# Attention in front of two expert layers: the output turned back a pair later in the score banks, and q, k and v loaded over all partitions at once

## The chip, the cores and the metric

One core of one Trainium2 chip runs the whole program in one launch. The metric is the device time of that launch in microseconds, as the median of several runs.

## What is computed

Attention with a learned position bias feeds a mixture of experts and then a gated feed-forward layer. Only the attention matters here:

```python
B, H, S, D = 4, 8, 576, 64
scores = scale * np.matmul(q, k.transpose(0, 1, 3, 2))
x = (np.log1p(np.abs(rel)) / psi_i)[..., None]      # rel = pos_i - pos_j
bias = np.maximum(x @ w1 + b1, 0.0) @ w2            # one value per head, i, j
scores = scores + bias.transpose(2, 0, 1)[None]
attn = np.exp(scores - np.max(scores, axis=-1, keepdims=True))
attn = attn / (np.sum(attn, axis=-1, keepdims=True) + 1e-09)
out = np.matmul(attn, v)
```

The rows of `out` (tokens x 512) then go through `_moe_ref` (8 experts, one per token) and `_moe2_ref`.

## The kernel before

**Stages.** A bias stage computes the bias table (`bias_stage`, up to about 62 us) and stores it to HBM. The attention follows (`front_stages`, to about 364 us), then routing, experts and the feed-forward layer, which the change doesn't touch.

**Pairs and slots.** Attention runs over NPAIR = 16 pairs of heads, pair p having batch p % 4 and head pair p // 4. The 576 query rows of a pair are cut into five slots: 0 to 3 hold 128 rows of either head (two units, h = 0 and 1), and slot 4 (`MIX`) the last 64 rows of both heads in one unit. That is nine units a pair. Each unit passes TensorE (`scores`, line 428, 4 matmuls of 288 columns, 8 for slot 4), VectorE (`add_bias`, line 587, with the row maximum), ScalarE (`exps`, line 653, with the row sum), and VectorE again (`turn`, line 597, a transpose into `pt`). The score banks are `s_ps`, two banks for each h, so the scores of one slot wait for the adds of the slot before (`s_b`).

**The sums.** `values` (line 535) multiplies `pt` by v on TensorE. It needs every transpose of its pair, so it runs one pair later. Its 18 blocks of keys are dealt over slots 0 to 3 of the following pair by `VISITS` (3, 5, 5 and 5 blocks, 16 matmul passes each), behind the scores that TensorE computes one slot ahead. They accumulate in four banks, `o_ps`.

**Out again.** In slot 4 ScalarE copies the sums to `ot` (`keep_out`, line 663, signals `s_oe`), and TensorE multiplies them back to rows = tokens and by the gate weights (`turn_back`, line 556, ten matmul passes, signals `s_bk`). Its output lies in `back_ps`, which are the first two banks of `o_ps`. VectorE divides by the row sums (`normal`, line 614, twice a pair, writes `a_xp`, signals `s_x`) in slot 0 of the next pair. So the next sums, which overwrite these banks, wait for `s_x` (line 542). GpSimd adds the gate logits (`add_logits`, line 499) after `normal`, and SyncE stores the tokens (`store_first`, `store_second`).

**Queues.** All loads and stores here go through SyncE, in written order: q and k of pair p + 2 (`load_qk`), the stores of pair p - 2, new bias tiles in each fourth pair, v of pair p + 1. In pair 0 v of pairs 0 and 1 stands behind q and k of pair 2. q and k must be twice in SBUF (partitions 0 to 63 and 64 to 127), v four times (every 32 partitions), so `load_qk` makes 4 loads and `load_v` 4, each from the same source rows. GpSimd splits q and k of a coming pair in two parts (`split_k`, `split_q`) as soon as the scores that use the same buffer are done. In the bias stage `loads` (line 389) issues q and k of pair 1 in steps 22 and 24.

Of the kernel before, what the change touches and what calls it, by code (L numbers as in the profile page):

```python
# [26 lines left out]
TPP = 9  # L27
# [248 lines left out]
def front_stages(sem, arena, psum, qt, kt, vt, ww, wg, biasd, xd, ident, rt, small):  # L276
# [6 lines left out]
    NG, NK = P // Q, S // Q  # L283
    VISITS = (range(0, 3), range(3, 8), range(8, 13), range(13, NK))
    pt = arena.at("a_pt", [P, 2, NK, 2 * P + Q], arena.PT)
# [19 lines left out]
    o_ps = psum[:, 4:8, :]  # L305
    back_ps = [psum[:, 4, :], psum[:, 5, :]]
    s_init, s_bias = sem("a_init"), [sem(f"a_bias{t}") for t in range(SLOTS)]
# [6 lines left out]

    def load_qk(e, pair, u, halves=(0, 1)):
        for half in (slice(64 * i, 64 * i + 64) for i in halves):
            e.dma_start(qraw[half, u, :, :].rearrange("p a s -> p (a s)"),
                        qt[bass.ds(pair, 1), :, :, :].rearrange("a p h s -> p (a h s)")).then_inc(s_q[u], 16)
            e.dma_start(kraw[half, u, :], kt[bass.ds(pair, 1), :, :].rearrange("a p s -> p (a s)"))\
                .then_inc(s_k[u], 16)  # L320

    def load_v(e, pair, u):
        for g in range(NG):
            e.dma_start(vv[Q * g:Q * g + Q, u, :, :].rearrange("p k d -> p (k d)"),
                        vt[bass.ds(pair, 1), :, :].rearrange("a p n -> p (a n)")).then_inc(s_v[u], 16)

# [9 lines left out]
    def set_constants(e):  # L336
        for u in range(2):
            e.memset(qs[:, u, S:640].bitcast(f32), 0.0).then_inc(s_init, 1)
        e.memset(xw[:, :, :, 64:XW], 0.0).then_inc(s_init, 1)
        for h in range(2):  # L340
            e.tensor_copy(xw[:, :, h, 0:64], ident[:, 64 * h:64 * h + 64].unsqueeze(1).to_broadcast([P, H // 2, 64]))\
                .then_inc(s_init, 1)
        e.wait_ge(s_init, sem.at(s_init, 5))
        e.wait_ge(s_k[0], sem.at(s_k[0], 32))
        e.tensor_copy(khi[:, 0, :], kraw[:, 0, :]).then_inc(s_sp, 1)
        e.wait_ge(s_q[0], sem.at(s_q[0], 32))
        e.tensor_copy(both(0, slice(0, P)), qraw[:, 0, :, :]).then_inc(s_qh, 1)
# [9 lines left out]
    def split_k(e, it, u):  # L357

        pair = it * 2 + u
        e.wait_ge(s_k[u], sem.at(s_k[u], it * 32 + 32))  # L360
        sem.apart(e, it)
# [13 lines left out]
    def split_q(e, it, u):  # L375

        pair = it * 2 + u
        e.wait_ge(s_q[u], sem.at(s_q[u], it * 32 + 32))
        sem.apart(e, it)
# [9 lines left out]
    def loads(e, step):  # L389

        if step in (2, 4, 6, 8):
            small(e, step // 2 - 1)
        if step in (22, 24):
            load_qk(e, 1, 1, (step // 2 - 11,))
        if step in (28, 30):
# [32 lines left out]
    def scores(e, p, u, uses, s, h):  # L428

        unit = p * TPP + 2 * s + h  # L430
        if s == 0 and h == 0:
            split_done(e, p)
        e.wait_ge(s_b, sem.at(s_b, unit if s == 0 and h == 0 else unit - 2 if s == 0 else unit - 1))
        parts = [(0, BLK), (1, S)] if s == MIX else [(h, 704 * h + P * s)]
# [11 lines left out]
    def sync(e):  # L446
# [18 lines left out]
        def pair(p, u, uses):  # L465
            def next_bias(slots):
                if not isinstance(p, int) and u == 1:
                    with e.If(uses % 2 == 1):
                        for s in slots:
                            e.wait_ge(s_b, sem.at(s_b, p * TPP + min(2 * s + 2, TPP)))  # L470
                            sem.apart(e, p)
                            load_bias(e, (p // B + 1) % (H // 2), s)
            next_bias((0,))
            if not (isinstance(p, int) and p >= NPAIR - 2):
                split_done(e, p)
                load_qk(e, p + 2, u)
            if isinstance(p, int) and p == 0:
                load_v(e, 0, 0)
                load_v(e, 1, 1)
            if from_pair(p, 2):  # L480
                store_first(p - 2, u)
                store_second(p - 2, u)
            next_bias(range(1, SLOTS))
            if from_pair(p, 1) and not (isinstance(p, int) and p == NPAIR - 1):
                e.wait_ge(s_o, sem.at(s_o, p))
                sem.apart(e, p)
                load_v(e, p + 1, 1 - u)

        each_pair(e, pair)
# [43 lines left out]
    def tensor(e):  # L533

        def values(p, u, uses, blocks):

            if blocks[0] == 0:
                e.wait_ge(s_v[u], sem.at(s_v[u], (uses + 1) * NG * 16))
                e.wait_ge(s_t, sem.at(s_t, p * SLOTS + SLOTS))
                sem.apart(e, p)  # L540
                if from_pair(p, 1):
                    e.wait_ge(s_x, sem.at(s_x, p * 2))
                    sem.apart(e, p)
# [12 lines left out]
        def turn_back(p):  # L556

            e.wait_ge(s_oe, sem.at(s_oe, p + 1))
            if isinstance(p, int) and p == 0:
                e.wait_ge(s_wg, sem.at(s_wg, 32))  # L560
# [7 lines left out]
        def pair(p, u, uses):  # L568
            for s in range(SLOTS):
# [3 lines left out]
                if exists(np_) and ns != MIX:  # L573
                    scores(e, np_, nu, nuses, ns, 1)
                if s != MIX and from_pair(p, 1):
                    values(p - 1, 1 - u, uses - 1 + u, VISITS[s])
                if s == MIX and from_pair(p, 1):
                    turn_back(p - 1)

        each_pair(e, pair)  # L580
        last = NPAIR - 1
        values(last, 1, NPAIR // 2 - 1, range(NK))
        turn_back(last)

    def vector(e):
# [42 lines left out]
        def pair(p, u, uses):  # L628
            for s in range(SLOTS):
# [3 lines left out]
                if exists(np_) and ns != MIX:  # L633
                    add_bias(np_, nu, nuses, ns, 1)
                if s == 0 and from_pair(p, 2):
                    for half in range(2):
# [1191 lines left out]
```

## Time and profile before

| what | us |
|---|---|
| median of 3 runs | 1098.96 (1096.1 to 1109.04) |
| profiled execution | 1099.54 |
| its span in the profile | 1097.7 |
| TensorE busy | 1014.5 (92% of the span) |
| VectorE busy | 793.3 (72%) |
| ScalarE, GpSimd busy | 411.2, 204.8 |
| mean granted TensorE clock | 0.963 of 2.4 GHz |

Rows of the view by stretch give: the stretch; its length; busy time of PE (TensorE matmuls), PEld (its weight loads), DVE (VectorE), ACT (ScalarE) and POOL (GpSimd), each with its count of instructions; the granted TensorE clock; the mean busy share of the DMA engines; GB/s. Rows of the timeline give: start, duration, engine, line, operation, output <- inputs, and in brackets the idle time before it with what ended it; SPq is SyncE's queue of DMA issues. Rows of waits give: who waited <- for whom: total us, how often, the longest. A matmul's own duration contains its way through the array, and matmuls overlap; how many start in a stretch tells the rate.

### The profile page before, as it was taken

The page shows a single profiled execution, that of the slowest core. Times are in us where ns is not written, and L with a number is a line of the kernel's source. Part 1 is how long each engine was busy: PE and PEld are TensorE (multiplying, and loading weights), DVE is VectorE, ACT ScalarE, POOL GpSimd, SP SyncE. Part 2 cuts the span into 40 slices and gives each one's busy share as a digit, 9 for nine tenths or more (in the row PEclk, how much of TensorE's full clock was granted, in tenths as well). Part 3 has the DMA queues.
Part 4 walks back from the last instruction along what each step waited for, and adds up shares of the span by engine and source line. Part 5 has one row for each costly group of instructions (what it writes and reads, how often), then busy time and mean ns, then how long its engine had stood idle before and what let it go on. Part 6 is the DMA issues. An engine that isn't in the chain of part 4 may idle for free.

```text
span 1097.7 us, 28662 instructions
## 1 busy us (share of the span) xinstructions
PE 1014.5 (92%) x10409; PEld 921.0 (84%) x10410; DVE 793.3 (72%) x1268; ACT 411.2 (37%) x783; POOL 204.8 (19%) x195
## 2 busy tenths in 40 slices
PE   5867778898888999999999999999999999999997
PEld 2346666676777899999999999999999999999996
DVE  8974768777787654774747479878777777777775
ACT  7863444444454334654434244221221212212111
POOL 2044243525360141221212000001010000100101
PEclk9987899989999889999999999999999999999999
DMA  4886688977963573561612170002000100100000
GB/s 148 288 230 141 146 208 170 235 152 160 227 151 67 168 240 117 191 205 61 203 50 88 60 258 2 1 0 80 29 29 0 45 12 0 57 0 0 30 1 29
DMA packets 68078, 117.43 MB, mean 107 GB/s; under 512 B 28384, under 2 KB 39696, under 8 KB 65984
## 3 DMA queue, kind: packets, MB, share of 16 engines
q1 hardware_dynamic: 64000, 103.45, 34.2%
q0 software_dynamic: 4032, 13.37, 3.8%
q8 instruction: 28, 0.46, 0.2%
q14 instruction: 18, 0.15, 0.0%
HBM read 91.41 MB, written 25.40 MB: 106 GB/s over the span
## 4 chain that ended last, share of the span: by engine, by line
PE 84%; issue 4%; DVE 3%; DMA 3%; ACT 3%; DVEq 1%; SPq 0%; ACTq 0%; POOL 0%; POOLq 0%
PE psum L1700 27%; PE psum L1708 13%; PE psum L1213 10%; PE psum L1222 10%; PE psum L551 10%; PE psum L438 8%; DMA bias_ihj<-b_res 2%; PE psum L563 2%; PE psum L1199 1%; DVE a_xp L624 1%; DMA a_v<-v 1%; PE psum L843 1%; ACT b_hid L234 1%; ACT a_ot L667 1%; ACT b_res L244 1%
## 5 line engine op out<-in xcount | busy, mean ns | idle before, releaser
L1655 DVE RECIPROCAL f_eg<-f_eg 128x384 f32<-128x384 f32 x72 | 183.3, 2546 | 0.0
L659 ACT ACTIVATE a_pr<-a_sc,a_nmax 128x576 f32<-128x576 f32 x144 | 110.9, 771 | 151.5 <-DVE a_nmax L593 151.0
L593 DVE CUSTOM_DVE_ANT_0 a_sc<-psum,a_bias 128x576 f32<-128x576 f32 x144 | 105.0, 755 | 75.2 <-PE psum L438 72.4
L551 PE MATMUL psum<-a_pt,a_v 32*64 32x128 f32 (+1 forms) x4608 | 108.8, 316 | 49.3 <-DVE a_xp L624 33.4
L1623 ACT ACTIVATE f_eg<-psum 128x384 f32<-128x384 f32 x72 | 35.4, 492 | 311.9 <-PE psum L1700 311.9
L1700 PE MATMUL psum<-f_x,f_ghi 128*128 (+1 forms) x576 | 147.5, 337 | 0.4 <-DVE f_x L1516 0.4
L1700 PE MATMUL psum<-f_x,f_vhi 128*128 (+1 forms) x576 | 146.1, 334 | 0.0
L551 PEld LDWEIGHTS psum<-a_pt,a_v 32*64 32x64 f32 x4608 | 87.7, 143 | 62.5 <-issue 57.1
L438 PE MATMUL psum<-a_khi,a_qs 128*128 128x288 f32 x320 | 107.7, 354 | 4.3 <-DVE a_nmax L593 4.2
L1700 PEld LDWEIGHTS psum<-f_x,f_ghi 128*128 128x128 f32 x576 | 105.8, 188 | 6.6 <-DVE f_x L1516 0.6
L1592 POOL DMA_INDIRECT out<-f_ob,f_cols x18 | 18.1, 1006 | 465.0 <-ACT f_ob L1609 316.3
L1700 PEld LDWEIGHTS psum<-f_x,f_vhi 128*128 128x128 f32 x576 | 104.0, 188 | 0.0
L605 DVE STREAM_TRANSPOSE a_pt<-a_pr 128x576 f32<-128x576 f32 x144 | 103.9, 756 | 0.0
L438 PE MATMUL psum<-a_klo,a_qs 128*128 128x288 f32 x320 | 98.0, 324 | 0.0
L1700 PE MATMUL psum<-f_x,f_glo 128*128 (+1 forms) x288 | 97.1, 337 | 0.0
L1700 PE MATMUL psum<-f_x,f_vlo 128*128 (+1 forms) x288 | 96.2, 334 | 0.0
L1651 DVE TENSOR_SCALAR f_eg<-f_eg 128x384 f32<-128x384 f32 x72 | 26.4, 367 | 88.5 <-ACT f_eg L1623 88.5
L438 PEld LDWEIGHTS psum<-a_khi,a_qs 128*128 128x128 f32 x320 | 68.8, 215 | 22.9 <-issue 17.6
L1222 PE MATMUL psum<-e_hhi,e_w2hi 128*128 128x288 f32 x288 | 87.4, 303 | 0.0
L1213 PE MATMUL psum<-e_xhi,e_w1hi 128*128 128x288 f32 x288 | 86.7, 301 | 0.0
L1708 PE MATMUL psum<-f_ohi,f_alo 128*128 128x512 f32 x216 | 85.4, 396 | 0.0
L1708 PE MATMUL psum<-f_olo,f_ahi 128*128 128x512 f32 x216 | 85.3, 395 | 0.0
(235 smaller groups left out, 2162.7 us busy)
## 6 DMA issues: line engine op xcount, KB each, us to landing
a_v<-v SPq DMA_DIRECT2D x64, 288.0 KB, 5.4
e_raw<-ew SPq DMA_DIRECT2D x16, 1024.0 KB, 5.2
bias_ihj<-b_res SPq DMA_DIRECT2D x36, 288.0 KB, 2.8
a_qraw<-q SPq DMA_DIRECT2D x32, 288.0 KB, 7.4
a_kraw<-k SPq DMA_DIRECT2D x32, 288.0 KB, 8.1
a_bias<-bias_ihj SPq DMA_DIRECT2D x16, 576.0 KB, 6.2
xn_t<-e_yn SPq DMA_DIRECT2D x8, 576.0 KB, 3.1
x_tokens<-a_xp SPq DMA_DIRECT2D x64, 64.0 KB, 6.3
```

Of the source, the lines that this page charges most:

```text
L438: mm = e.matmul(s_ps[:, h, half, 0:HALF], qs[:, u, c:c + P], k[:, u, a * S + half * HALF:a * S + (half + 1) * HALF], start=(i == 0), stop= ...
L551: mm = e.matmul(o_ps[64 * h:64 * h + 64, g, to:to + n], vv[rows, u, k, 64 * h:64 * h + 64], pt[rows, u, k, first:first + n], start=(k == 0 ...
L593: e.tensor_tensor_reduce(sc[:, h, :].rearrange("p (a s) -> p a s", a=2), s_ps[:, h, :, 0:HALF], bias[:, 2 * s + h, :].rearrange("p (c s) - ...
L605: t = e.transpose(pt[:, u, :, at:at + Q], pr[:, w, S * h:S * h + S].rearrange("p (k q) -> p k q", q=Q))
L659: mm = e.activation(pr[:, w, S * h:S * h + S], sc[:, h, :], ACT.Exp, bias=nmax[:, h:h + 1], scale=-1.0, accum_out=sums[:, u, 2 * s + h:2 * ...
L1213: mm = e.matmul(bank[:, 0:BT], w[:, k, :], x[:, u, k, :], start=(k == 0 and n == 0), stop=(k == KD - 1 and n == 2))
L1222: mm = e.matmul(banks.y[:, k, 0:BT], w[:, k * P:(k + 1) * P], h[:, f % 3, :], start=(f == 0 and n == 0), stop=(f == KF - 1 and n == 2))
L1623: e.activation(self.eg[:, k % 2, :], self.g_ps[k % 2][:, 0:CHUNK], ACT.Exp, scale=-1.0).then_inc(self.s_e, 1)
L1651: e.tensor_scalar(x, x, 1.0, None, ALU.add).then_inc(self.s_c, 1)
L1655: e.reciprocal(x, x).then_inc(self.s_c, 1)
L1700: mm = e.matmul(acc[:, 0:CHUNK], a, b, start=(q == 0 and i == 0), stop=(q == KD - 1 and i == 2))
L1708: mm = e.matmul(self.o_ps[t], x, y, start=(f == 0 and i == 0), stop=(f == KFF - 1 and i == 2))
```

## The change

- `back_ps` moves from `o_ps` to the h = 1 score banks. `turn_back(p - 2)` runs in slot 3 of pair p, between the scores of slot 4 and the sums, no longer `turn_back(p - 1)` in slot 4. It waits also for `normal` of the pair before it and for the add of slot 3, h = 1. The last two turns stand behind the loop.
- `normal(p - 2)` moves on VectorE from slot 0 to slot 3 of pair p. The scores of slot 0, h = 1 of the next pair wait for it (`s_x`).
- `values` waits for ScalarE's copy (`s_oe`) in place of `s_x`.
- `VISITS` deals 5, 5, 5 and 3 blocks.
- q, k and v are replicated on the host, and each is one load over 128 partitions; the semaphores count 16 in place of 32 or 64. q and k of pair 1 are both issued in step 22.
- SyncE's order: v of pair 0 ahead of q and k of pair 2; the stores of pair p - 2 at the end of pair p, behind v and all bias tiles, and the bias tile of slot 4 behind v.

```diff
-    VISITS = (range(0, 3), range(3, 8), range(8, 13), range(13, NK))
+    VISITS = (range(0, 5), range(5, 10), range(10, 15), range(15, NK))
-    back_ps = [psum[:, 4, :], psum[:, 5, :]]
+    back_ps = [s_ps[:, 1, half, :] for half in range(2)]
-    def load_qk(e, pair, u, halves=(0, 1)):
-        for half in (slice(64 * i, 64 * i + 64) for i in halves):
-            e.dma_start(qraw[half, u, :, :].rearrange("p a s -> p (a s)"),
-                        qt[bass.ds(pair, 1), :, :, :].rearrange("a p h s -> p (a h s)")).then_inc(s_q[u], 16)
...
+    def load_qk(e, pair, u):
+        e.dma_start(qraw[:, u, :, :].rearrange("p a s -> p (a s)"),
+                    qt[bass.ds(pair, 1), :, :].rearrange("a p n -> p (a n)")).then_inc(s_q[u], 16)
+        e.dma_start(kraw[:, u, :], kt[bass.ds(pair, 1), :, :].rearrange("a p n -> p (a n)")).then_inc(s_k[u], 16)
     def load_v(e, pair, u):
-        for g in range(NG):
-            e.dma_start(vv[Q * g:Q * g + Q, u, :, :].rearrange("p k d -> p (k d)"),
-                        vt[bass.ds(pair, 1), :, :].rearrange("a p n -> p (a n)")).then_inc(s_v[u], 16)
+        e.dma_start(vv[:, u, :, :].rearrange("p k d -> p (k d)"),
+                    vt[bass.ds(pair, 1), :, :].rearrange("a p n -> p (a n)")).then_inc(s_v[u], 16)
@@ loads @@
-        if step in (22, 24):
-            load_qk(e, 1, 1, (step // 2 - 11,))
+        if step == 22:
+            load_qk(e, 1, 1)
@@ scores @@
+        if s == 0 and h == 1 and from_pair(p, 3):
+            e.wait_ge(s_x, sem.at(s_x, p * 2 - 4))
@@ sync, pair @@
             next_bias((0,))
+            if isinstance(p, int) and p == 0:
+                load_v(e, 0, 0)
             if not (isinstance(p, int) and p >= NPAIR - 2):
                 split_done(e, p)
                 load_qk(e, p + 2, u)
             if isinstance(p, int) and p == 0:
-                load_v(e, 0, 0)
                 load_v(e, 1, 1)
-            if from_pair(p, 2):
-                store_first(p - 2, u)
-                store_second(p - 2, u)
-            next_bias(range(1, SLOTS))
+            next_bias(range(1, MIX))
             if from_pair(p, 1) and not (isinstance(p, int) and p == NPAIR - 1):
                 e.wait_ge(s_o, sem.at(s_o, p))
                 sem.apart(e, p)
                 load_v(e, p + 1, 1 - u)
+            next_bias((MIX,))
+            if from_pair(p, 2):
+                store_first(p - 2, u)
+                store_second(p - 2, u)
@@ values @@
                 if from_pair(p, 1):
-                    e.wait_ge(s_x, sem.at(s_x, p * 2))
+                    e.wait_ge(s_oe, sem.at(s_oe, p))
@@ turn_back @@
             e.wait_ge(s_oe, sem.at(s_oe, p + 1))
+            e.wait_ge(s_x, sem.at(s_x, p * 2))
+            e.wait_ge(s_b, sem.at(s_b, min((p + 3) * TPP - 1, NPAIR * TPP) if isinstance(p, int) else (p + 3) * TPP - 1))
@@ tensor, pair @@
+                if s == MIX - 1 and from_pair(p, 2):
+                    turn_back(p - 2)
                 if s != MIX and from_pair(p, 1):
                     values(p - 1, 1 - u, uses - 1 + u, VISITS[s])
-                if s == MIX and from_pair(p, 1):
-                    turn_back(p - 1)
...
         last = NPAIR - 1
+        turn_back(last - 1)
         values(last, 1, NPAIR // 2 - 1, range(NK))
         turn_back(last)
@@ vector, pair @@
-                if s == 0 and from_pair(p, 2):
+                if s == MIX - 1 and from_pair(p, 2):
                     for half in range(2):
                         normal(p - 2, u, uses - 1, half)
@@ kernel @@
-        "q": np.ascontiguousarray(qp), "k": np.ascontiguousarray(kp.reshape(NPAIR, D, 2 * S)), "v": np.ascontiguousarray(vp),
+        "q": np.tile(qp.reshape(NPAIR, D, 2 * S), (1, 2, 1)), "k": np.tile(kp.reshape(NPAIR, D, 2 * S), (1, 2, 1)), "v": np.tile(vp, (1, 4, 1)),
```

## Rows read from the trace of the kernel before

**Rows 1.** Busy time by stretch: pair 1, pair 3, eleven pairs, two single pairs.

```profile
83.24:107.94 24.70, 18.90 (x338) 16.14 (x339) 12.39 (x28) 8.37 (x21) 10.19 (x6) 0.76 0.60 131
...
129.65:151.15 21.50, 14.22 (x338) 11.92 (x339) 13.92 (x32) 8.33 (x22) 8.10 (x6) 1.00 0.93 251
...
151.15:339.85 188.70, 160.76 (x3719) 138.25 (x3718) 150.28 (x342) 91.92 (x231) 82.11 (x69) 0.92 0.77 176
...
184.89:200.75 15.86, 13.41 (x338) 11.51 (x338) 13.46 (x32) 8.26 (x21) 7.61 (x5) 1.00 0.76 161
...
218.51:237.29 18.78, 16.31 (x339) 14.09 (x339) 13.72 (x32) 8.41 (x22) 7.62 (x5) 0.83 0.73 156
```

**Rows 2.** Waits from 151.15 to 339.85 us.

```profile
POOL a_khi L367 <- PE psum L438: 87.2, 10, 10.5
DVE a_sc L593 <- PE psum L438: 36.4, 53, 2.1
...
PE psum L551 <- DVE a_xp L624: 27.7, 12, 2.7
```

**Rows 3.** Timeline around the start of the sums of one pair.

```profile
198.29 0.29 PE L438 MATMUL psum<-a_klo,a_qs 128*128 128x288 f32 x1
...
199.64 0.96 DVE L624 TENSOR_TENSOR a_xp<-psum,a_rinv 128x288 f32<-128x288 f32 x2
...
200.75 1.70 PE L551 MATMUL psum<-a_pt,a_v 32*64 32x160 f32 x48 [2.17 <-DVE a_xp L624]
...
202.79 0.44 PE L438 MATMUL psum<-a_klo,a_qs 128*128 128x288 f32 x1
```

**Rows 4.** Timeline of slots 2 to 4 of that pair.

```profile
206.14 0.40 PE L438 MATMUL psum<-a_khi,a_qs 128*128 128x288 f32 x1
...
207.17 0.76 DVE L593 CUSTOM_DVE_ANT_0 a_sc<-psum,a_bias 128x576 f32<-128x576 f32 x1 [0.19 <-PE psum L438]
...
207.40 1.64 PE L551 MATMUL psum<-a_pt,a_v 32*64 32x160 f32 x80
...
207.85 0.75 DVE L593 CUSTOM_DVE_ANT_0 a_sc<-psum,a_bias 128x576 f32<-128x576 f32 x1
...
208.97 0.40 PE L438 MATMUL psum<-a_khi,a_qs 128*128 128x288 f32 x1
...
210.57 0.76 DVE L593 CUSTOM_DVE_ANT_0 a_sc<-psum,a_bias 128x576 f32<-128x576 f32 x1 [0.61 <-PE psum L438]
...
212.34 0.60 ACT L667 ACTIVATE a_ot<-psum 128x512 f32<-128x512 f32 x1
...
213.46 1.49 PE L563 MATMUL psum<-a_xw,a_ot 128*128 x10 [0.28 <-ACT a_ot L673]
...
214.69 0.39 PE L438 MATMUL psum<-a_khi,a_qs 128*128 128x288 f32 x1
```

**Rows 5.** Busy time by stretch: q, k, v loads; bias tile loads.

```profile
70.00:83.00 13.00, 7.00 (x26) 5.82 (x24) 9.90 (x23) 5.91 (x14) 4.54 (x3) 0.63 1.01 225
...
207.50:211.50 4.00, 4.00 (x164) 3.62 (x168) 3.39 (x9) 1.68 (x5) 0.95 (x1) 1.00 1.09 331
```

**Rows 6.** Timeline: v of pairs 0 and 1, and the first sums.

```profile
71.90 4.12 SPq L324 DMA_DIRECT2D a_v<-v  x8
...
76.91 0.77 DVE L605 STREAM_TRANSPOSE a_pt<-a_pr 128x576 f32<-128x576 f32 x1
...
83.24 1.91 PE L551 MATMUL psum<-a_pt,a_v 32*64 32x160 f32 x48 [4.89 <-DMA a_v<-v]
```

**Rows 7.** Timeline: a stall in pair 1; a copy in the bias stage.

```profile
95.25 0.81 PE L551 MATMUL psum<-a_pt,a_v 32*64 32x128 f32 x9 [3.00 <-issue]
...
51.49 0.74 ACT L244 ACTIVATE b_res<-psum,b_invp 128x576 f32<-128x576 f32 x1 [1.85 <-DMA bias_ihj<-b_res]
```

**Rows 8.** DMA issues of the page: count, KB each, us to landing.

```profile
a_kraw<-k SPq DMA_DIRECT2D x32, 288.0 KB, 8.1
```

**Rows 9.** Groups by line, 151.15 to 339.85 us: busy us, mean ns.

```profile
L370 POOL TENSOR_TENSOR a_klo<-a_kraw,a_khi 128x1152 fp32r<-128x1152 f32 x10 | 26.5, 2650 | 1.8 <-POOL a_khi L367 1.8
```

More of the change, by code:

```diff
@@ L313, in front_stages @@
         sem.loop("a_" + n) for n in ("s", "b", "e", "t", "o", "oe", "bk", "r", "x"))
-    def load_qk(e, pair, u, halves=(0, 1)):
-        for half in (slice(64 * i, 64 * i + 64) for i in halves):
-            e.dma_start(qraw[half, u, :, :].rearrange("p a s -> p (a s)"),
-                        qt[bass.ds(pair, 1), :, :, :].rearrange("a p h s -> p (a h s)")).then_inc(s_q[u], 16)
-            e.dma_start(kraw[half, u, :], kt[bass.ds(pair, 1), :, :].rearrange("a p s -> p (a s)"))\
-                .then_inc(s_k[u], 16)
+    def load_qk(e, pair, u):
+        e.dma_start(qraw[:, u, :, :].rearrange("p a s -> p (a s)"),
+                    qt[bass.ds(pair, 1), :, :].rearrange("a p n -> p (a n)")).then_inc(s_q[u], 16)
+        e.dma_start(kraw[:, u, :], kt[bass.ds(pair, 1), :, :].rearrange("a p n -> p (a n)")).then_inc(s_k[u], 16)
     def load_v(e, pair, u):
-        for g in range(NG):
-            e.dma_start(vv[Q * g:Q * g + Q, u, :, :].rearrange("p k d -> p (k d)"),
-                        vt[bass.ds(pair, 1), :, :].rearrange("a p n -> p (a n)")).then_inc(s_v[u], 16)
+        e.dma_start(vv[:, u, :, :].rearrange("p k d -> p (k d)"),
+                    vt[bass.ds(pair, 1), :, :].rearrange("a p n -> p (a n)")).then_inc(s_v[u], 16)
     def load_bias(e, hp, s):
@@ L343, in set_constants @@
         e.wait_ge(s_init, sem.at(s_init, 5))
-        e.wait_ge(s_k[0], sem.at(s_k[0], 32))
+        e.wait_ge(s_k[0], sem.at(s_k[0], 16))
         e.tensor_copy(khi[:, 0, :], kraw[:, 0, :]).then_inc(s_sp, 1)
-        e.wait_ge(s_q[0], sem.at(s_q[0], 32))
+        e.wait_ge(s_q[0], sem.at(s_q[0], 16))
         e.tensor_copy(both(0, slice(0, P)), qraw[:, 0, :, :]).then_inc(s_qh, 1)
@@ L359, in split_k @@
         pair = it * 2 + u
-        e.wait_ge(s_k[u], sem.at(s_k[u], it * 32 + 32))
+        e.wait_ge(s_k[u], sem.at(s_k[u], it * 16 + 16))
         sem.apart(e, it)
@@ L377, in split_q @@
         pair = it * 2 + u
-        e.wait_ge(s_q[u], sem.at(s_q[u], it * 32 + 32))
+        e.wait_ge(s_q[u], sem.at(s_q[u], it * 16 + 16))
         sem.apart(e, it)
@@ L537, in values @@
             if blocks[0] == 0:
-                e.wait_ge(s_v[u], sem.at(s_v[u], (uses + 1) * NG * 16))
+                e.wait_ge(s_v[u], sem.at(s_v[u], (uses + 1) * 16))
                 e.wait_ge(s_t, sem.at(s_t, p * SLOTS + SLOTS))
```

## The prediction

> **What bounds the kernel now.** I read the page first, for the stages and the lines that cost most. The change touches only the attention part, from about 60 to 364 us, so the argument is about that part. The busy time by stage comes next, cut where the value sums of each pair start. In 151.15 to 339.85 us, eleven pairs, TensorE is busy 160.8 of 188.7 us and VectorE 150.3: nearly level, and neither is full; their mean clock is 0.92 [rows 1]. One pair costs 188.7 / 11 = 17.15 us on average. Pairs differ by clock: one with a granted clock of 1.00 took 15.86 us, one with 0.83 took 18.78 [rows 1]. The waits of the same stretch name the gap: TensorE's value sums waited 27.7 us in 12 places, 2.3 us a pair, for VectorE's write of a_xp (line 624, `normal`) [rows 2]. VectorE itself waits 36.4 us for scores, so it has slack too, and GpSimd waits 87.2 us, 8.7 a pair [rows 2]. The timeline shows the gap in one pair: the last score matmul starts at 198.29, `normal` runs from 199.64, the sums begin at 200.75 after 2.17 us of idle TensorE, and right behind this gap a score matmul takes 0.44 us where it took 0.29 before it: the clock fell to the half level [rows 3].
>
> **Part 1: sums wait for the copy alone.** The back-turn's output leaves banks 4 and 5, so the sums of pair p need only ScalarE's copy of pair p-1 (`s_oe`). That copy follows the end of the sums by 0.5 us and takes about 1 us (from 212.34 in this pair) [rows 4], while the sums are some 3 us away behind 16 score matmuls. The 2.3 us wait goes. What is late next has to be walked, since VectorE is nearly full.
>
> Steps, all at clock 1.00 [rows 4]: a group of 8 score matmuls to the sums behind it 1.26 us (206.14 to 207.40), to another group some 0.2 less, 1.05; 80 sums 1.57 (207.40 to 208.97), 48 sums about 1.05; ten back-turn matmuls 1.2 (213.46 to 214.69); scores to the first bias add 1.03 (206.14 to 207.17), for the one unit of slot 4 1.60 (208.97 to 210.57); adds 0.68 apart (207.17 to 207.85); two transposes 1.36 (VectorE's 13.46 us of a pair [rows 1] less 9 adds, `normal` and 0.3 of reciprocals, over 9, twice); the two `normal`s 0.96 [rows 3].
>
> **Part 2: the back-turn a pair later, in the score banks.** It moves from slot 4 to slot 3, between the scores of slot 4 and 48 sums. Its input was copied a pair ago, so the wait for `s_oe` (about 0.3 us of idle now) is gone. Its new wait, for the add of slot 3 half 1, ends some 0.7 us before it is asked, because the slot 4 scores (1.26 us) stand in front. `normal` moves on VectorE behind the slot 4 add. Behind it stand the transposes of slot 3 (nobody needs them for 3 us) and the first add of the next pair. The scores of the next pair's second half now wait for `normal` (`s_x`); it ends about as the first half starts, 0.5 us before the second half is asked.
>
> Walk, 0 being where TensorE starts the next pair's slot 0: VectorE is still busy until 1.0, first add at 1.03, second 1.71, transpose of slot 4 from 2.39 to 3.1. TensorE has issued slot 0 by 1.05 and waits for the first add: slot 1 scores at about 1.95 (a new idle of 0.9 us that the back-turn covered before), second half 2.6, sums of slot 0 (80 now) 3.3 to 4.9, slots 1 and 2 with 1.26 + 1.57 each to 10.5, slot 4 scores to 11.75, back-turn to 12.95, 48 sums to 14.1. VectorE: slot 4 add at 12.1, `normal` 12.8 to 13.8, transposes to 15.15, which is 1.0 into the next pair: the walk closes at 14.2 us. The floors lie just below: VectorE has 9 adds (6.1), 9 transposes (6.2), `normal` 0.9, reciprocals 0.3 = 13.5 us. The same walk for the kernel before gives 15.9 against 15.86 measured [rows 1], so I add only 0.1: 14.3 us at clock 1.00, a gain of 1.55 a pair, not 2.3.
>
> **The clock.** A pair of 17.15 us on average against 15.86 at clock 1.00 loses 1.3 us to stretches at the half level (1.2 GHz) [rows 1]. The idle of 2.17 us before them becomes 0.9 plus two pauses of 0.1 to 0.2. I take it that three quarters of this loss go: the average pair is then 14.3 + 0.3 = 14.6. Eleven pairs: 11 x (17.15 - 14.6) = 28 us. With no such gain it is 11 x 1.55 = 17 us; with all of it 31.
>
> **Part 3: loads over all partitions.** Bytes stay the same: 4 loads of 288 KB for v and 4 for q and k a pair become 3 of 1.18 and 0.59 MB. SyncE issues 3 instead of 8 at some 0.5 us, 2.5 us saved on a queue with room. The rate: the q, k and v loads of 70 to 83 us move 225 GB/s with the engines full, the bias loads over 128 partitions 331 [rows 5]. So between none and a third of the transfer time is saved. In a steady pair it is hidden either way: a pair moves about 2.6 MB (161 GB/s x 15.86 us [rows 1]), 11.4 us at 225 GB/s, and each load has a pair's time to land. It is worth 0 there. The Trainium skill, "SBUF — State Buffer", section on the DMA port swizzle, has 64 partitions reach only half of the ports (196 against 328 GB/s at 1 MiB); this agrees with these two windows, and by it the v load takes about 3.6 us.
>
> **Part 4: v of pair 0 first in the queue.** Now SyncE issues it from 71.90, behind four q and k loads, and TensorE waits 4.89 us, until 83.24, while the last transpose that the sums need starts at 76.91 and ends at 77.68 [rows 6]. Issued at 69.3, 1.18 MB at even 225 GB/s take 5.2 us, with 2 us around it 76.6, before TensorE is free (83.24 - 4.89 = 78.35). The whole 4.9 us go.
>
> **First pairs, end, other queues.** 83.24 to 151.15, three pairs of 24.7 to 21.5 us [rows 1], takes 67.9 us, with stalls that no semaphore explains, 3.00 us in the first [rows 7]; I keep them. Two waits for `normal` there (some 2.3 each) go and pair 1 loses its back-turn (1.5), but the new wait stands against them and a half clock stays in places: -6 us. At the end pair 15 gains a back-turn (+1.2) and values(15) no longer waits for `normal` (-1.0): 0. Bias stage: q and k of pair 1 come as one burst at step 22; a copy waits 1.85 us for a store queued behind these loads now [rows 7]; I take -0.5, bounds +1 and -2. SyncE's stores now stand at the end of a pair and delay the next q and k issue to about 4.5 us into it; with today's landing of 8.1 us [rows 8] they are there at 13.5. GpSimd is held at `add_logits` until `normal` of slot 3 is done: its split starts 2.6 us later, at 15, takes two subtractions of 2.65 us [rows 9] and two casts of about 1.1, some 8 with the pauses, and ends at 23 where it is needed at 28.5. Cost 0 while that slack of 5 us holds.
>
> Sum: -28 - 4.9 - 6 + 0 - 0.5 = -39.4 us. The profiled execution took 1099.5 us (span 1097.7), 0.6 above the median shown: 1099.5 - 39.4 = 1060.1, or 1059.6 against the median. I say 1060.
>
> **Rivals.** (a) The clock is not given back: half-clock stretches stay as they are. For it: they may depend on the whole mix of small pieces, and the slot boundary still has pauses. Then 17 + 4.9 + 4 = 26: 1073. Chance 0.2. (b) VectorE or TensorE doesn't keep the walk: VectorE would be 95% busy, and each handover that runs 0.3 us late five times a pair costs 1.5 us, which eats the gain; what stays is pair 0's v and a little clock: 1085. Chance 0.1. (c) The other side: TensorE gets the half clock more often, because the scores of slots 0 and 1 now come in four short pieces with pauses. A pair at 0.83 took 18.78 us and one at 1.00 15.86 [rows 1], so 0.1 of mean clock costs 1.7 us. A pair of 14.3 is back at 17.15 when its mean clock is 0.83 (now 0.92); at 0.75 it costs 18.6, 11 x 1.4 = 16 us more than now, and less the 9 of the start the kernel takes 1107. Against it: the pauses are shorter than today's. Chance 0.03. (d) Slower by the queue: q and k behind the stores. It decides only if landing takes 18 us instead of 8, then each us costs 15 us in all. Chance 0.02.
>
> **Numbers.** The forecast's own range, 1049 to 1068, has 0.65. The low end takes all of the clock, 14.1 a pair and stalls of the first pairs partly covered; reaching into (a) gives 1049 to 1078 for 8 in 10. Two per cent, about what can be told from no change, is 22 us: below 1077 lies the forecast, (a) nearly whole, 0.85; within 2% 0.12; slower 0.03.
>
> **What would show it.** TensorE has no wait for L624 before the sums; it has waits of about 0.9 us before score matmuls for VectorE's add; pairs of 14.2 to 14.8 us with clock above 0.95; VectorE above 13 us of each; the first sums near 78.4 us; q, k, v packets at over 300 GB/s; GpSimd waits for `normal` and not for scores. It is wrong if pairs stay above 15.5 at clock 1.00 (the walk), if clock stays at 0.9 (the clock step), or if TensorE waits for `a_ql` or a DMA at a pair's start (the queues).

## The result, and the profile after

| | us |
|---|---|
| before, median of 4 runs | 1100.96 (1096.1 to 1109.04) |
| changed, median of 4 runs | 1048.57 (1046.72 to 1052.59) |
| ratio, with its 95% interval | 0.952 (0.946 to 0.959) |
| span of the changed kernel's profile | 1046.9 (before: 1097.7) |

The direction was as forecast, and so was the mechanism in the steady pairs; but the gain is 52 us where 39 were forecast, and the time lies 0.4 us under the low end of the range (1049). The surplus comes from the first three pairs, for a reason that the forecast hadn't.

Busy time by stretch of the changed kernel, cut like [rows 1] where the sums of a pair start: pairs 1, 2 and 3, then eleven pairs. Columns as before.

```profile
80.53:94.39 13.86, 12.84 (x329) 10.61 (x329) 12.06 (x30) 8.27 (x21) 11.65 (x7) 0.99 0.51 192
94.39:113.04 18.65, 15.61 (x338) 13.10 (x339) 14.04 (x32) 8.33 (x21) 6.27 (x5) 0.91 0.35 125
113.04:129.11 16.07, 14.09 (x339) 11.75 (x339) 13.66 (x32) 8.38 (x22) 8.57 (x6) 1.00 0.91 313
129.11:288.06 158.95, 149.14 (x3719) 128.06 (x3719) 149.61 (x342) 91.14 (x230) 86.35 (x70) 1.00 0.64 211
```

Eleven pairs take 158.95 us where [rows 1] have 188.70, 14.45 a pair, at a granted clock of 1.00 where it was 0.92. Pair 1 takes 13.9 us where it took 24.7.

Waits of the changed kernel in its steady pairs, 131.46 to 290.57 us:

```profile
POOL r_part L508 <- DVE a_xp L628: 65.9, 11, 6.6
...
PEld psum L437 <- DVE a_nmax L597: 10.3, 11, 1.0
...
PE psum L437 <- DVE a_nmax L597: 7.8, 11, 0.7
...
POOL a_khi L364 <- PE psum L437: 2.0, 5, 0.4
```

The wait of the sums for a_xp, 27.7 us in [rows 2], is gone. In its place stand eleven waits of TensorE for VectorE's first add of a slot 0: 0.7 us a pair for its matmuls, 0.9 for its weight loads. GpSimd waits for `normal` (now line 628), not for scores.

The start of the attention, where [rows 6] and [rows 7] have a wait of 4.89 us for v and a copy that waits 1.85 us; and the stalls of pairs 2 and 3. Timeline of the changed kernel:

```profile
80.53 1.73 PE L552 MATMUL psum<-a_pt,a_v 32*64 32x160 f32 x80
...
55.12 0.74 ACT L244 ACTIVATE b_res<-psum,b_invp 128x576 f32<-128x576 f32 x1 [4.55 <-DMA bias_ihj<-b_res]
...
100.72 0.96 PE L552 MATMUL psum<-a_pt,a_v 32*64 32x128 f32 x30 [2.08 <-issue]
...
124.52 0.77 PE L552 MATMUL psum<-a_pt,a_v 32*64 32x128 f32 x23 [1.02 <-issue]
```

Nothing waits for v. The copy in the bias stage waits 4.55 us, so the attention begins later. And the stalls without a releaser before the sums, up to 3.0 us each before, are 2.08 and 1.02.

Below, "the stalls" of a kernel are all waits of TensorE's matmuls without a releaser (`<-issue`) of 0.3 us or more in pairs 1 to 3, added up: 9.95 us before (3.00, 2.37, 2.40 and 2.18) and 3.1 in the changed kernel. Pauses of 0.2 us, which every steady pair of the changed kernel has too, are not counted; some of the texts written before a run count them or set the stalls of the changed kernel at 4.1 to 4.5.

**The ledger.** As marks I use the nine-column reciprocal of VectorE (`inverse`), which every pair has once in slot 0, so that all kernels can be cut alike:

| stretch | before | changed | moved | forecast |
|---|---|---|---|---|
| to the mark of pair 1 | 80.4 | 82.7 | +2.3 | -0.5 |
| three pairs | 71.6 | 48.8 | -22.9 | -10.9 (v 4.9, rest 6) |
| eleven pairs | 188.9 | 159.1 | -29.8 | -28 |
| the rest | 756.7 | 756.3 | -0.4 | 0 |
| sum | | | -50.8 | -39.4 |

So most of the miss is in one row: 12 us too little in the first three pairs, and 2 in the eleven, with 3 us of the other sign in the bias stage. In the three pairs, cut as in [rows 1], TensorE's busy time fell from 50.0 to 42.5 us (1.4 of it the turn-back that pair 1 no longer has; granted clock 0.86 before, 0.96 after). The stalls fell by 6.9 us, and the rest is waits for v and for `normal`.

### The profile page after: what moved, and what is told of

Read it like the earlier page. It is cut to its first block, busy times and chain, and to the rows that moved or that the text cites. A ratio compares the mean times of both kernels' runs of the same rounds, so it can differ in the third digit from the quotient of the medians.

```text
span 1046.9 us, 28553 instructions
## 1 busy us (share of the span) xinstructions
PE 993.2 (95%) x10409; PEld 901.3 (86%) x10410; DVE 791.9 (76%) x1268; ACT 410.0 (39%) x783; POOL 203.8 (19%) x195
## 4 chain that ended last, share of the span: by engine, by line
PE 68%; DVE 2%; issue 1%; POOL 1%; ACT 1%; DMA 0%; POOLq 0%; DVEq 0%
PE psum L1704 28%; PE psum L1712 14%; PE psum L1217 11%; PE psum L1226 11%; PE psum L1203 1%; PE psum L552 1%; PE psum L437 1%; DVE f_eg L1659 0%; PE psum L1265 0%; PE psum L566 0%; DMA e_xin<-x_tokens,e_col 0%; PE psum L847 0%; DVE r_inq L962 0%; POOL e_xin L1169 0%; POOL e_col L1165 0%
## 5 line engine op out<-in xcount | busy, mean ns | idle before, releaser
L437 PE MATMUL psum<-a_khi,a_qs 128*128 128x288 f32 x320 | 101.1, 336 | 13.8 <-DVE a_nmax L597 13.8
L1596 POOL DMA_INDIRECT out<-f_ob,f_cols x18 | 18.2, 1009 | 464.9 <-ACT f_ob L1613 316.9
L552 PE MATMUL psum<-a_pt,a_v 32*64 32x128 f32 (+1 forms) x4608 | 98.9, 294 | 8.3 <-issue 8.3
L552 PEld LDWEIGHTS psum<-a_pt,a_v 32*64 32x64 f32 x4608 | 79.6, 131 | 20.1 <-issue 17.9
L437 PEld LDWEIGHTS psum<-a_khi,a_qs 128*128 128x128 f32 x320 | 62.4, 195 | 34.6 <-DVE a_nmax L597 17.9
L437 PE MATMUL psum<-a_klo,a_qs 128*128 128x288 f32 x320 | 90.9, 304 | 0.0
```

The costliest lines, as they stand in the source:

```text
L437: mm = e.matmul(s_ps[:, h, half, 0:HALF], qs[:, u, c:c + P], k[:, u, a * S + half * HALF:a * S + (half + 1) * HALF], start=(i == 0), stop= ...
L552: mm = e.matmul(o_ps[64 * h:64 * h + 64, g, to:to + n], vv[rows, u, k, 64 * h:64 * h + 64], pt[rows, u, k, first:first + n], start=(k == 0 ...
```

## Experiments: which part brings what

All kernels below start from the kernel before or from the changed one, and were timed beside the kernel before on the same chip; the ratio to it has a 95% interval where it is given. The chips differ from one group of kernels to another, so differences of medians between groups are good to a few microseconds only, and stalls come from one profile of each kernel.

**The turn-back alone.** From the changed kernel, the loads and v's place are put back:

```diff
-        e.dma_start(vv[:, u, :, :].rearrange("p k d -> p (k d)"), ...
+        for g in range(NG):
+            e.dma_start(vv[Q * g:Q * g + Q, u, :, :].rearrange("p k d -> p (k d)"), ...
...
-            if isinstance(p, int) and p == 0:
-                load_v(e, 0, 0)
...
```

> The turn-back part alone: banks, waits, block deal, place of the turn and of the stores as in the changed kernel; q, k and v still loaded in 4 + 4 pieces, v of pair 0 behind q and k of pair 2. Theory 1 (the first three pairs gained 19 us, 13 more than forecast, because TensorE no longer waits for v and so keeps its clock, and because stalls without a releaser depend on when the code is reached): steady pairs 14.5 us, the wait for v of 4.9 us and the slow clock of pair 1 stay, so first sums at about 83 us and pairs 1 to 3 about 58 to 60 us; time 1063 to 1068. Theory 2 (long packets of the old loads hold up the loading of code and the clock follows): the same 14.5 in the steady pairs where no code is loaded, but the stalls without a releaser in pairs 1 to 3 stay at 10 us; time also about 1065, told apart by these stalls.

Measured: 1069.93 us, ratio 0.970 (0.962 to 0.978), some 2 us above both theories. Three pairs take 65.4 us and not 58 to 60, eleven pairs 162.5 (14.8 each), then a last pair 17.3 us where the changed kernel has 13.1. The stalls stay, 10.3 us where the kernel before has 9.95. That is what theory 2 says: the turn-back leaves them alone. Its own -6 us in the first three pairs (71.6 to 65.4) are of the size of the forecast.

**The loads alone.** The kernel before with the new load form and nothing else:

```diff
-        for g in range(NG):
-            e.dma_start(vv[Q * g:Q * g + Q, u, :, :].rearrange("p k d -> p (k d)"), ...
+        e.dma_start(vv[:, u, :, :].rearrange("p k d -> p (k d)"), ...
...
```

> The kernel before with each of q, k and v as one load over 128 partitions (q and k of pair 1 both in step 22), nothing else. Theory 1: steady pairs unchanged at 17.1 us, the wait for v falls from 4.9 to about 1 us since the same bytes land at 330 instead of 225 GB/s, the bias stage is 2 us longer as in the changed kernel; stalls in pairs 1 to 3 stay near 10 us; time 1093 to 1098. Theory 2: the stalls fall from 10 to 3 us as in the changed kernel; time 1084 to 1089.

Measured: 1079.3 us, ratio 0.983 (0.974 to 0.991). By the ratio that is 19 us (10 to 28) less than before, by the medians 22 to 24; and it is 5 less than even theory 2 said. Busy time by stretch: its first three pairs, then its steady ones.

```profile
79.61:133.25 53.64, 43.89 (x1015) 37.53 (x1015) 41.29 (x94) 25.71 (x66) 28.62 (x17) 0.94 0.62 219
...
133.25:320.83 187.58, 159.63 (x3718) 137.44 (x3718) 150.27 (x342) 91.85 (x231) 82.16 (x69) 0.93 0.50 175
```

The steady pairs cost 17.05 us as before (17.15). Nearly all is won in the first three, 53.6 us for 67.9, and ahead of them, where the first sums start 3.6 us earlier. The wait of TensorE's first sums there (its timeline):

```profile
79.61 1.09 PE L548 MATMUL psum<-a_pt,a_v 32*64 32x160 f32 x48 [1.39 <-DMA a_v<-v]
```

That is 3.5 us of the 4.9 us wait for v, without moving v in the queue. The stalls fall to 1.8 us, at a pace of the pairs that is no faster than before. Theory 2 holds in this: the load form governs them. How it does so is the question of the next three kernels.

**v first, alone.** The kernel before, `load_v(e, 0, 0)` ahead of `load_qk` in pair 0.

> The kernel before with v of pair 0 issued ahead of q and k of pair 2, in the old pieces, nothing else. Theory 1: the wait of 4.9 us goes and pair 1 keeps more of its clock (24.7 us before, 20 to 21 after); time 1090 to 1093. Rival: only the wait goes, or the wait for v moves to q and k of pair 2, which come later: time 1096 to 1101.

Measured: 1096.1 us, ratio 0.9965 (0.992 to 1.001), so the time alone doesn't tell. The trace does: the first sums start at 77.93 us with no wait, the three pairs take 64.3 us (7.4 less), and the stalls are 10.7 us, one of them 4.5. So the wait went as forecast, and the stalls stayed with the old load form; the time is that of the rival. The three parts overlap: alone they take 6.3, 18.2 and 7.4 us from the three pairs, together 22.9.

**Why the load form matters to the stalls.** The trace lists instructions among the traffic of the core's 16 DMA engines, in packets of 16 KB on a queue of their own (28 of them in the kernel before). One of them is in the microsecond from 92 us of the kernel before, when the q, k, v transfers run dry (queue: packets, MB, share of the engines' time):

```profile
q8 instruction: 1, 0.02, 7.6%
```

It begins at 92.49 us and takes 1.22; TensorE stands still from 92.25 to 95.25 [rows 7]. In the changed kernel the packet that comes next after the bias stage begins at 85.09 us, and TensorE works on without a stall until 98.6. In the steady pairs, 170 to 260 us, no kernel's trace has an instruction packet, and such stalls don't occur there. The question is whether the code waits for the length of the data burst (theory L) or for single packets of data ahead of it (theory S). A packet of v, 9216 B, takes 656 ns on the average in the kernel before and 424 ns in the changed one; one of q or k, 4608 B, 297 and 213 ns.

Longer bursts, new form: v's first 16 blocks loaded a second time, into spare space.

```diff
+        e.dma_start(v_more[:, u, :, :].rearrange("p k d -> p (k d)"),
+                    vt[bass.ds(pair, 1), :, 0:(NK - 2) * P].rearrange("a p n -> p (a n)")).then_inc(s_v[u], 16)
```

> The changed kernel with 16 of v's 18 blocks loaded a second time into spare space behind each v load (1.05 MB more a pair, packets of 8192 B over all partitions, and the sums wait for both), so that the transfers in front of the code's packets last as long as in the kernel before while their shape stays the new one. Theory L (a code packet comes to its turn when the queued data ahead of it is gone, so the stalls follow the length of the bursts): the stalls without a releaser in pairs 1 to 3 rise from 4.5 to 8 to 11 us, pairs 1 to 3 take 54 to 58 us in place of 48.8; steady pairs, which load no code, stay at 14.4 to 14.8; time 1053 to 1060. Theory S (what matters is the time of a single packet, 656 ns in the old form against some 400): stalls stay below 5.5 us and the time below 1051.

Measured: 1055.91 us, ratio 0.962 (0.955 to 0.969), in the range of theory L. But the stalls are 5.4 us for 3.1, under the 8 to 11 of theory L, and three pairs take 52.0 us for 48.8 where it said 54 to 58. Steady pairs are 14.56 us for 14.46. The profiled execution, 1051.6 us, was the fastest of four. So longer bursts cost something, 2.3 us of it in stalls, and this kernel decides for neither theory.

Shorter packets, old form: each old load cut in two column halves.

```diff
         for g in range(NG):
-            e.dma_start(vv[Q * g:Q * g + Q, u, :, :].rearrange("p k d -> p (k d)"),
+            for c in range(2):
+                e.dma_start(vv[Q * g:Q * g + Q, u, 9 * c:9 * c + 9, :].rearrange("p k d -> p (k d)"),
...
```

> The kernel before with every load of q, k and v cut in two halves of its columns: same 32 or 64 partitions, same bytes, packets of 4608 and 2304 B in place of 9216 and 4608, twice as many loads. Theory L: the port or the engines stay as slow, the bursts as long, the stalls without a releaser in pairs 1 to 3 stay at 9 to 11 us, time 1096 to 1106. Theory S: single packets are half as long, the stalls fall to 5 us or less, time 1085 to 1092.

Measured: 1093.35 us, ratio 0.994 (0.991 to 0.998). Busy time by stretch while the first loads run, and the one stall that is left, in the timeline:

```profile
60.00:83.00 23.00, 14.77 (x72) 11.63 (x72) 16.93 (x39) 15.28 (x33) 12.07 (x10) 0.76 0.79 214
```

```profile
96.31 0.81 PE L553 MATMUL psum<-a_pt,a_v 32*64 32x128 f32 x9 [3.52 <-issue]
```

The rate is as low as in [rows 5] and the wait for v as long (4.79 us), so the bursts are as long. The packets of v now take 294 ns, and the stalls fall from 9.95 to 3.5 us, which speaks for theory S. But they fall by the three of pairs 2 and 3. The stall of pair 1, in front of the same nine matmuls as in [rows 7], is 3.52 us where it was 3.00, and its instruction packet begins at 93.56 us, again in the microsecond in which the data run dry: this one was not helped by shorter packets, as theory L says. The time, too, lies between the two theories; the three pairs (65.1 us) kept their slow clock (0.84). So neither theory holds for all stalls.

Shorter packets, new form, on top of the better bias stage shown below:

> The changed kernel with q and k of pair 1 at the start (e4_qk1_early) and every load of q, k and v cut in two column halves, still over all 128 partitions: packets of 4608 and 2304 B at the new rate, some 200 and 100 ns each. Theory S (the code's packets wait behind single packets of data): the stalls without a releaser in pairs 1 to 3 fall from 4.1 to 1 to 2.5 us, pairs 1 to 3 from 47.8 to 44 to 46 us, time 1 to 4 us below e15_early_again. Theory M (below some 400 ns a packet no longer counts; what is left of the stalls is the distance from one code packet to the next): stalls stay at 3.5 to 4.5, no difference beyond 1 us.

Measured: 1043.87 us (1040.83 to 1045.25), beside 1042.3 for the same kernel with whole packets; stalls 3.6 us beside 2.5. Packets of v take 211 ns in place of some 420, and nothing is won: that is theory M, as far as the new form goes.

Shown is, then, that the load form decides: stalls of 9.95, 10.3 and 10.7 us with the old one in whole packets, 0 to 5.4 with the new one. By which way is open: size and number of the packets, the rate and the length of the burst all change with it. When TensorE gets to a piece of code counts as well: the kernel below that makes the sums wait in each pair has the new loads and no stall at all in pairs 1 to 3. The 2 to 5 us that are left in the others are not explained by any run, and differences of a microsecond between single profiles carry no weight.

## Experiments: the steady pairs and the clock

**The wait put back.** In the changed kernel the sums wait again for VectorE, now for its transposes of slot 0, which stand about where `normal` stood:

```diff
                     e.wait_ge(s_oe, sem.at(s_oe, p))
                     sem.apart(e, p)
+                if not isinstance(p, int) or p < NPAIR - 1:
+                    e.wait_ge(s_t, sem.at(s_t, p * SLOTS + SLOTS + 1))
+                    sem.apart(e, p)
```

> The changed kernel, but the sums wait again for VectorE in slot 0: for the transposes of slot 0 of the following pair, behind two adds and in the place where `normal` stood (1.4 us of VectorE in place of 1.0). This gives the wait of 2.2 to 2.7 us back without moving anything. Theory A (this wait was the cost, and it also pulled the clock down): TensorE waits some 2.5 us a pair before the sums, granted clock of the steady pairs falls from 1.00 to 0.90 to 0.97, and pairs take 16.5 to 17.5 us; time 1076 to 1092. Theory B (the clock depends on the mix, not on this gap): clock stays at 1.00, pairs take 15.8 to 16.4; time 1065 to 1075.

Measured: 1107.62 us, ratio 1.007 (1.004 to 1.010): this wait alone costs more than the whole change brought. Busy time of eleven pairs, waits of the same stretch, and the timeline after one such wait:

```profile
137.69:346.48 208.79, 170.25 (x3718) 146.43 (x3719) 150.50 (x341) 91.72 (x231) 84.18 (x70) 0.86 0.50 160
...
PE psum L555 <- DVE a_pt L612: 30.9, 11, 2.9
```

```profile
156.10 2.98 PE L555 MATMUL psum<-a_pt,a_v 32*64 32x160 f32 x80 [2.73 <-DVE a_pt L612]
...
159.41 0.44 PE L437 MATMUL psum<-a_klo,a_qs 128*128 128x288 f32 x1
...
161.18 1.64 PE L555 MATMUL psum<-a_pt,a_v 32*64 32x160 f32 x80
```

The wait is 2.8 us a pair. A pair takes 18.98 us and not 14.5 + 2.8: behind the wait the 80 sums take 2.98 us in place of 1.64 and score matmuls start 0.24 us apart in place of 0.13, the half level (1.2 GHz), until about 161 us. So a wait of 2.8 us costs 4.5. This is theory A, and more than its upper end of 17.5 us a pair, which had only the mean clock of the kernel before in it. Here the clock falls behind each of the eleven waits. In the kernel before, the wait for `normal` was 2.0 to 2.7 us, and the clock fell behind nine of twelve. Its length doesn't say which: the two longest, 2.70 and 2.67 us, left the clock up, and the shortest, 1.98 us, didn't. The longest, in the timeline of the kernel before:

```profile
151.15 1.07 PE L551 MATMUL psum<-a_pt,a_v 32*64 32x160 f32 x48 [2.70 <-DVE a_xp L624]
...
152.53 0.29 PE L438 MATMUL psum<-a_khi,a_qs 128*128 128x288 f32 x1
```

**Which engine sets the pair.** Two kernels with work left out, of which only the length of the pairs is read:

```diff
-            ops = [(a, c, k) for a, c in parts for k in (khi, klo)]
+            ops = [(a, c, k) for a, c in parts for k in ((khi, klo) if s == 0 else (khi,))]
```

> The changed kernel without the low part of k in the scores of slots 1 to 4 (16 of 40 score matmuls a pair left out, 2.1 us of TensorE), to see which engine sets a steady pair. If VectorE is the bound, pairs stay at 14.1 to 14.5 us; if TensorE is, they fall to 12.4 to 12.9; if both in turn as in the walk, about 13.7. Only the length of the pairs is read, since what comes behind depends on values that this changes.

```diff
-                t = e.transpose(pt[:, u, :, at:at + Q], pr[:, w, S * h:S * h + S].rearrange("p (k q) -> p k q", q=Q))
+                n_k = NK if p_first(p) else NK // 2
+                t = e.transpose(pt[:, u, 0:n_k, at:at + Q], pr[:, w, S * h:S * h + n_k * Q].rearrange("p (k q) -> p k q", q=Q))
```

> The changed kernel with only the first half of each transpose from pair 2 on (some 3 us of VectorE a pair left out), the other side of the same question. If VectorE is the bound, pairs fall to about 13.3 us, where TensorE's own work ends it; if TensorE is, they stay at 14.4. Only the length of the pairs is read.

Measured, by the marks: 13.2 to 13.4 us in most pairs without these scores (13.5 on the average of ten), and 14.1 to 14.4 (mean 14.2) with half transposes, against 14.46. Each kernel ran once. Busy time of ten pairs of the first and eleven of the second:

```profile
144.16:279.60 135.44, 119.59 (x3236) 97.92 (x3243) 132.03 (x312) 82.98 (x210) 77.40 (x66) 0.97 0.69 227
```

```profile
129.57:285.50 155.93, 148.27 (x3719) 127.50 (x3718) 121.32 (x342) 91.58 (x232) 84.56 (x70) 1.00 0.66 214
```

2.6 us of VectorE less a pair (149.6 to 121.3 us over eleven pairs) gains 0.3 us; 2.1 us of TensorE less gains 0.9 (1.1 in most pairs), and then VectorE is busy 132.0 of 135.4 us. So TensorE sets the pair, and VectorE stands about 1 us behind it. The 0.7 us wait of TensorE for the first add is not a wait for a busy VectorE: it is the way score, add, next score, and it stays with half transposes.

## Experiments: the bias stage, and a faster version

**q and k of pair 1 at the start.** In the changed kernel the copy behind step 22 waits 4.55 us. Both loads go to the start of the stage, where the DMA engines are busy 38% of the first 10 us and then idle until the first store at 13 us:

```diff
-        if step == 22:
-            load_qk(e, 1, 1)
...
-                              {"first loads": lambda e: load_qk(e, 0, 0), "loads": loads,
+                              {"first loads": lambda e: (load_qk(e, 0, 0), load_qk(e, 1, 1)), "loads": loads,
```

> The changed kernel with q and k of pair 1 issued right behind those of pair 0 at the start of the bias stage, where the DMA engines are idle until the first store at 13 us, in place of step 22. In the changed kernel one copy of the bias stage waits 4.55 us for a store queued behind these two loads (kernel before: 1.85 and 1.1 in two places). If those loads are the cause, the bias stage ends 4 to 5 us earlier, at about 60.5 us in place of 65, and the time is 1043 to 1045. Rival: the stage's stores fill the DMA engines anyway, and the waits stay at other steps; time 1048.

Measured: 1043.17 us (1042.75 to 1043.54), ratio 0.9475 (0.941 to 0.954). The first mark stands at 78.1 us in place of 82.7, and no copy waits more than 0.2 us for a store. All of the 5 us came.

**The two loads two steps apart.** q in step 22, k in step 24:

> The changed kernel with q of pair 1 in step 22 and k of pair 1 in step 24, each still one load over 128 partitions. If the burst of 1.18 MB in one step makes the stage 2.3 us longer than before, half of it goes: first score add of the attention at about 63 us in place of 64.3, time 1046 to 1047. Rival: the wait comes from the fence of all stores ahead of the bias tile of step 26 and any load ahead of it costs the same: no change, 1048.5.

Measured: 1045.93 us (1045.69 to 1046.99); the first mark is at 80.9, and the copies wait 3.1 us in four places, none over 1.3. So the burst in one step cost 2 us of its own, and any load in that stretch the rest.

**Sums in slot 4.** The wait for the first add can be filled. On top of the kernel with the early loads, one block of sums in slot 4, and then two (the edit shown):

```diff
-    VISITS = (range(0, 5), range(5, 10), range(10, 15), range(15, NK))
+    VISITS = (range(0, 5), range(5, 10), range(10, 14), range(14, 16), range(16, NK))
...
-                if s != MIX and from_pair(p, 1):
+                if from_pair(p, 1):
```

> The changed kernel with q and k of pair 1 at the start (as e4_qk1_early, 1043.2 us) and the last of the 18 blocks of sums moved from slot 3 to slot 4, behind the scores of the next pair's slot 0, where TensorE waits 0.7 to 1.0 us a pair for VectorE's first add. The block takes about 0.35 us and fills part of that wait; the copy by ScalarE starts later but is not asked for another 1.5 us. Expected: pairs 14.1 to 14.3 in place of 14.55, time 1037 to 1041. Rival: the scores of half 1 then wait for `normal`, or the sums for the copy, and nothing is gained: 1043.

> The same with two blocks in slot 4 and two in slot 3 (5, 5, 4, 2, 2). By the walk the wait for the first add is filled whole, but the sums of the next pair start only when the copy is done, about 1.6 us behind the last block, where the scores between last 1.3: pairs 13.9 to 14.2, time 1035 to 1040. Rival: VectorE, 13.5 us busy a pair, sets the pace with its order, and the time equals that of e11_one_block_slot4 within 2 us.

Measured: 1044.15 us (1042.74 to 1047.36) with one, 1041.37 (1041.1 to 1042.34) with two; both expectations were missed. With one, the steady pairs are 14.27 us by the marks, as expected, but the three pairs take 50.1 us for 47.8 and the last one 15.0 for 13.0, and nothing is gained. With two, the steady pairs take 14.07 us, 0.4 less, some 4 us in all. Part of it is lost again near the end: the last pair takes 15.2 us in place of 13.0, by a stall without a releaser, in the timeline of the kernel with two blocks:

```profile
284.70 1.82 PE L550 MATMUL psum<-a_pt,a_v 32*64 32x128 f32 x39 [2.42 <-issue]
```

With half packets as well, beside the kernel with the early loads on the same chip:

> Both at once: two blocks of sums in slot 4 (e12_two_blocks_slot4) and half packets over all partitions. If the parts add up, 2 us from the blocks and what e13_early_half_packets gains: 1036 to 1041; rival: the stall near the end of the loop (2.4 us in e12_two_blocks_slot4) stays and the time is within 1 us of 1041.

> e4_qk1_early unchanged, on the same chip as the two beside it, so that one or two microseconds between them can be told: 1042 to 1044.

Measured: 1039.96 us (1039.5 to 1041.63) and 1042.3 (1042.06 to 1042.69). The ratios to the kernel before are 0.946 (0.937 to 0.954) and 0.9475 (0.939 to 0.956). The fastest version is 2.3 us under its neighbour, about 9 under the changed kernel (timed on another chip), and its four runs lie wholly below the neighbour's. The half packets have no share in it that can be told.

## Why the prediction was right and where it failed

- **The wait of the sums.** Right: it went, and the turn-back part alone brought 33 us (ratio 0.970).
- **The walk.** 14.3 us at clock 1.00 were forecast, 14.45 measured. The pause of TensorE in front of slot 1 was given as 0.9 us and is 0.7 to 0.9. The floors were read well: VectorE's 13.5 us is about where the pairs stop (13.2 to 13.4) when TensorE has less to do, and it lies 1 us below the pair, which TensorE sets.
- **The clock.** The step was right, its size too small: three quarters of 1.3 us a pair were taken, all of it came (1.00). Together with the walk, whose 14.3 us was 0.15 too short, the steady term is 29.8 for 28; that it came so near is in part two errors of opposite sign. And the reason given, that the idle of 2.17 us shrinks, holds for this change as a whole (the wait put back brought the half level back), though the length of a wait doesn't decide it.
- **v first.** Right: no wait for v, in the changed kernel and alone.
- **Loads over all partitions, "worth 0 there".** "There" is a steady pair, and there the 0 was right at the old pace (17.05 us for 17.15); at the new pace the old form costs 3.4 us in eleven pairs, with waits for a bias tile and for k. What failed is that the sum has no term for the load form anywhere else: alone it brings some 20 us, and about as much, with v's place, on top of the turn-back, nearly all in the first three pairs. The waits of VectorE and GpSimd of the turn-back alone, 146.65 to 309.17 us:

```profile
POOL a_khi L367 <- DMA a_kraw<-k: 8.3, 2, 4.2
...
DVE a_sc L599 <- DMA a_bias<-bias_ihj: 5.2, 4, 1.6
```

- **"Stalls that no semaphore explains: I keep them."** This step failed, and most of the miss lies in it: they were carried over without a reason. They depend on the form of the loads, and fell from 9.95 to 3.1 us. With them and the wait for v went the half level of the first pairs (0.76 and 0.84 to 0.99 and 0.91), for which the sum had no term either: TensorE's busy time in the three pairs is some 6 us less by it. The -6 us given for these pairs is what the turn-back brings alone (-6.3). The 12 missing come with the load form, as the kernel with the loads alone shows; how they divide between stalls and clock isn't shown by a run of its own.
- **The bias stage.** -0.5 with bounds +1 and -2; measured +2.3, outside. The burst was seen, but its cost was weighed against the wait there was (1.85 us), not against the fence: SyncE waits in step 26 for earlier stores to land before it issues the bias tile, and some of them stand behind 1.18 MB. In the changed kernel it has issued the last store by 50.3 us and the tile only at 55.03 (before: 49.4 and 51.40); its timeline:

```profile
55.03 0.34 SPq L331 DMA_DIRECT2D a_bias<-bias_ihj  x1
```

- **GpSimd and the stores.** Right: GpSimd waits for `normal`, 6 us a pair, and nobody for GpSimd.

## What to carry to other kernels

Read the stalls without a releaser in a trace against the DMA packets of that moment: where code is still being loaded, as in the pairs before a loop and its first pass, the form of the data loads beside it can be worth more than the length of their transfers. Don't carry such stalls over as a constant. A wait of TensorE is worth more than its length when the clock falls behind it, here 4.5 us for 2.8, so it is to be removed first. And look for idle time of the DMA engines (here before the first store at 13 us) before putting a load into a stretch in which stores pace the work.

## What was not expected of the hardware

- A packet of v, 9216 B, took 656 ns in loads over 32 partitions and 424 ns over 128; the changed kernel's stretch from 80 to 83 us moved 415 GB/s, where [rows 5] have 225. The Trainium skill, "SBUF — State Buffer", section on the DMA port swizzle, has 32 or 64 partitions reach 8 of the 16 ports and 128 all of them; these two rates agree with it.
- Loads over 128 partitions in place of 32 and 64, and nothing else, took the stalls in code loading from 9.95 to 1.8 us. Halving packets in the old form, at an unchanged rate, took away three of the four and left that of pair 1 (3.52 us). The Trainium skill, "Runtime: NRT & Kernel Launch", section "Instruction fetch mechanics", calls the cost of a new block of code mostly hidden. These traces agree for the kernels with the new loads (0 to 5.4 us in three pairs) and not for those with the old ones in whole packets (some 10 us).
- The half level came behind each of the eleven waits of 2.7 to 2.9 us in the kernel with the wait put back, and ended 3 to 6 us after them. Behind the waits of 0.7 us in the changed kernel's steady pairs it never came; with the turn-back alone it came once there, at 217 us, where no wait of its matmuls was over 1.2 us. In the kernel before it came behind nine of twelve waits of 2.0 to 2.7 us, and not behind the two longest.
